# Routing into fixed visits: an expert's first 512 tokens keep their own visit, one-hot rows are built column by column, and the first visit is transposed tile by tile

## What is computed

```python
def _moe_ref(x, w_gate, w_noise, noise, w1, w2):      # N, D, E, F = 1536, 320, 8, 1024
    logits = x @ w_gate
    noise_scale = np.log1p(np.exp(x @ w_noise))
    noisy_logits = logits + noise_scale * noise
    top2 = np.argpartition(-noisy_logits, 2, axis=1)[:, :2]
    ...                                                # top2_w: softmax over the two
    for e in range(E):
        for k in range(2):
            mask = top2[:, k] == e
            h = np.maximum(x[mask] @ w1[e], 0.0)
            out[mask] += top2_w[mask, k, None] * (h @ w2[e])
```

## Time and profile before

| | before |
|---|---|
| median of 3 runs | 757.9 us |
| lowest, highest | 757.38, 763.17 us |
| profiled execution | 757.65 us |
| its span, first to last instruction | 755.5 us |
| mean granted clock of PE | 0.955 of full |
| PE busy | 680.6 us, 90% |
| DVE, ACT, POOL busy | 400.1, 286.8, 107.8 us |
| `h_hi` steps (line 545) | 160: 20 visits of 8 steps, 8 in layer 1, 12 in layer 2 |

### The profile page before, as it was taken

How to read it: one execution, slowest core, us unless ns; L and a number is a source line. 1 busy time by engine, 2 the same in 40 slices (tenths; PEclk the granted TensorE clock), 3 DMA queues, 4 the chain that set the end, 5 groups by cost and what they waited for, 6 DMA issues and landing times.

```text
span 755.5 us, 11010 instructions
## 1 busy us (share of the span) xinstructions
PE 680.6 (90%) x4020; PEld 610.9 (81%) x4021; DVE 400.1 (53%) x615; ACT 286.8 (38%) x466; POOL 107.8 (14%) x134
## 2 busy tenths in 40 slices
PE   2999953598999999999739999999999999999997
PEld 2889722598899898898638899898888888889887
DVE  7677549565445465365335545554554554444522
ACT  6644250245444354354214343343342332333311
POOL 4333204710201201200060200101200001000000
PEclk9999885699999999999959999999999999999999
DMA  7667660775445455450146352443432423513000
GB/s 209 147 146 171 191 242 10 196 225 156 150 122 153 131 161 159 127 158 35 37 153 189 105 154 63 126 126 107 144 97 84 125 83 108 150 60 95 0 0 35
DMA packets 32565, 93.11 MB, mean 123 GB/s; under 512 B 4848, under 2 KB 14832, under 8 KB 32528
## 3 DMA queue, kind: packets, MB, share of 16 engines
q1 hardware_dynamic: 25040, 76.23, 34.8%
q0 software_dynamic: 3264, 11.15, 5.6%
q10 hardware_dynamic: 4224, 5.24, 1.9%
HBM read 79.49 MB, written 13.11 MB: 123 GB/s over the span
## 4 chain that ended last, share of the span: by engine, by line
PE 86%; DVE 7%; issue 2%; DMA 2%; ACT 1%; POOL 1%; DVEq 0%; ACTq 0%; POOLq 0%
PE pY L1073 12%; PE pY L1074 12%; PE pY L1075 12%; PE pH L1060 10%; PE pH L1061 9%; PE pH L1062 9%; PE pH L1065 5%; PE pH L1063 5%; PE psS L918 3%; PE psYa L971 3%; PE pT L1041 2%; PE psYa L984 1%; PE psF L1005 1%; PE psD L928 1%; PE pT L1042 1%
## 5 line engine op out<-in xcount | busy, mean ns | idle before, releaser
L545 ACT ACTIVATE h_hi<-pH 128x512 fp32r<-128x512 f32 x160 | 95.8, 599 | 292.9 <-PE pH L1065 292.9
L811 DVE SCALAR_TENSOR_TENSOR h_lo<-pH,h_hi 128x512 fp32r<-128x512 f32 x160 | 110.5, 691 | 177.2 <-ACT h_hi L545 176.1
L1073 PE MATMUL pY<-w_hi,h_hi 128*128 128x320 f32 x608 | 188.9, 311 | 3.0 <-DVE h_lo L811 2.6
L1074 PE MATMUL pY<-w_lo,h_hi 128*128 128x320 f32 x608 | 187.5, 308 | 0.0
L1075 PE MATMUL pY<-w_hi,h_lo 128*128 128x320 f32 x608 | 187.5, 308 | 0.0
L1060 PE MATMUL pH<-x_hi,w_hi 128*128 128x512 f32 (+2 forms) x324 | 128.4, 396 | 9.2 <-issue 5.7
L1061 PE MATMUL pH<-x_lo,w_hi 128*128 128x512 f32 (+2 forms) x324 | 124.7, 385 | 0.0
L1062 PE MATMUL pH<-x_hi,w_lo 128*128 128x512 f32 (+2 forms) x324 | 124.2, 383 | 0.0
L1073 PEld LDWEIGHTS pY<-w_hi,h_hi 128*128 128x128 f32 x608 | 114.1, 188 | 12.1 <-issue 5.7
L645 DVE TENSOR_TENSOR w_lo<-stage,w_hi 128x1024 fp32r<-128x1024 f32 (+1 forms) x80 | 108.5, 1358 | 25.6 <-ACT w_hi L491 25.5
L1074 PEld LDWEIGHTS pY<-w_lo,h_hi 128*128 128x128 f32 x608 | 114.1, 188 | 4.2
(11 more groups left out here) (184 smaller groups left out, 625.5 us busy)
## 6 DMA issues: line engine op xcount, KB each, us to landing
stage<-in_w SPq DMA_DIRECT2D x40, 640.0 KB, 3.9
stage<-in_w SPq DMA_DIRECT2D x40, 512.0 KB, 3.6
stage<-in_w SPq DMA_DIRECT2D x40, 256.0 KB, 3.9
results_by_slot<-acc ACTq DMA_DIRECT2D x8, 640.0 KB, 3.7
qk<-in_qk_t SPq DMA_DIRECT2D x16, 240.0 KB
kv<-in_kv_n SPq DMA_DIRECT2D x8, 480.0 KB
results_by_slot<-acc SPq DMA_DIRECT2D x6, 640.0 KB, 9.4
og<-in_o_n SPq DMA_DIRECT2D x2, 960.0 KB, 9.4
```

Of the source, the lines that this page charges most:

```text
L545: act.activation(HH[s % 2][:, :], pH[s % 2][:, :], ACT.Relu).then_inc(hh_done[layer], 1)
L811: dve.scalar_tensor_tensor(out=HL[s % 2][:, :], in0=pH[s % 2][:, :], scalar=0.0, in1=f32(HH[s % 2][:, :]), op0=ALU.max, op1=ALU.subtract). ...
L1073: pe.matmul(y[:, 0:XD], hh, wh, start=(f == 0), stop=False)
L1074: pe.matmul(y[:, 0:XD], hh, wl, start=False, stop=False)
```

## The change

- **Fixed visits.** Expert e's first 512 tokens go to visit e. Only what exceeds 512 goes to spare visits (`OVER` = 6 of them). Every choice gets a position `at` = 2048 e + rank (`SPAN`), and e x 2048 enters by a third matmul (`bases`) added to `psU`. The plan of the spare visits, and `rowid` for them, `dest` and the counts, are computed after the first 8 visits' `rowid`.
- **Tile and place.** `hi`, the tile's first position, is `at` rounded by adding and subtracting a large number; `lo` is the rest.
- **One-hot by column.** For each of the 24 columns DVE makes `in_row` (128 elements) and the tile-id half of `ids` (32 elements), with a scalar per lane; POOL makes the other half (32 elements) likewise. PE sums groups of 4.
- **Spare visits.** 24 more matmuls (`psO`, 48 columns) give the spare visits' rows. They stand in PE's queue behind the first tile's transposes and wait for `over_picked`.
- **First visit.** Each tile of it has a semaphore (`xin_first`) and is transposed as it lands, into six banks in two halves; ACT and DVE work by halves, and `up` of the first step waits for each round by itself.
- **Weights.** ACT's first `split_hi` moves ahead of its `xT` copies, DVE's `split_lo` of pieces 0 to 3 ahead of the logits; piece 4 stays behind `rowid`. SP loads the weights of visits 1 to 7 by a fixed number. Seven matmuls of 512 columns replace the 32 of 128 whose results nobody reads.

```diff
-            pool.wait_ge(rt_reached, 1)
-            for k in range(2):
-                ...
-                    pool.tensor_tensor(reached_id[:, at, n, :], reached[:, at, :], ...
+            pool.wait_ge(rt_where, 1)
+            for n in range(2 * NT):
+                pool.tensor_scalar(ids[:, n, 1, :], row_of[:, :, :].rearrange("p e t -> p (e t)"), hi[:, n // NT, n % NT:n % NT + 1], lane[:, 0:1],
+                                   ALU.is_equal, ALU.mult).then_inc(rt_lanes, 1)
 ...
+            split_hi(0, 0, 0, range(PIECES))
             for t in range(1, NT, 2):
 ...
             act.activation(e2[:, :], dl[:, :], ACT.Exp).then_inc(rt_e2, 1)
-            split_hi(0, 0, 0, range(PIECES))
 ...
+            split_lo(0, 0, 0, (0, 1, 2, 3))
             dve.wait_ge(rt_ln, 1)
 ...
+            rlink(dve.tensor_tensor_scan(line(incl), reset96[:, :], psU, 0.0, ALU.mult, ALU.add))
+            rlink(dve.tensor_tensor(line(pos), psR, line(incl), ALU.add))
+            for k in range(2):
+                ins = dve.tensor_tensor(d8[:, k, :, :], oh[:, k, :, :], pos[:, :, :].rearrange("p e t -> p t e"), ALU.mult)
+            rlink(ins)
 ...
+            rlink(dve.tensor_reduce(flat24(at), d8[:, :, :, :].rearrange("p k t e -> p (k t) e"), AX.X, ALU.add))
+            rlink(dve.tensor_scalar(flat24(hi), flat24(at), -(P - 1) / 2, TO_TILE, ALU.add, ALU.add))
+            rlink(dve.tensor_scalar(flat24(hi), flat24(hi), TO_TILE, None, ALU.subtract))
+            rlink(dve.tensor_tensor(flat24(lo), flat24(at), flat24(hi), ALU.subtract))
+            dve.sem_inc(rt_where, 1)
+            for n in range(2 * NT):
+                k, t = n // NT, n % NT
+                dve.tensor_scalar(in_row[:, n, :], iotaP[:, :], lo[:, k, t:t + 1], None, ALU.is_equal)
+                dve.tensor_scalar(ids[:, n, 0, :], row_of[:, :, :].rearrange("p e t -> p (e t)"), hi[:, k, t:t + 1], float(t),
+                                  ALU.is_equal, ALU.mult).then_inc(rt_place, 1)
+            dve.wait_ge(rt_inv, 1)
+            rlink(dve.tensor_copy(part[:, :], psI[:, MR:2 * MR]))
+            dve.scalar_tensor_tensor(out=rowid[:, 0:MR], in0=psI[:, 0:MR], scalar=float(P), in1=part[:, :], op0=ALU.mult, op1=ALU.add).then_inc(rt_rows, 1)
+            split_lo(0, 0, 0, (4,))
 ...
+            dve.tensor_scalar(over_ids[:, :, 1, :], over_in[:, :, :], lane[:, 0:1], None, ALU.mult).then_inc(over_picked, 1)
 ...
-            pe.matmul(psU, ones[:, :], rows, start=True, stop=True).then_inc(rt_rank, 1)
+            pe.matmul(psU, ones[:, :], rows, start=True, stop=False)
+            pe.matmul(psU, ones[:, :], bases[:, :], start=False, stop=True).then_inc(rt_rank, 1)
 
             for n in range(2 * NT):
                 if n % INV == 0:
-                    pe.wait_ge(rt_place, n // INV + 1)
-                if n % NT == 0:
-                    pe.wait_ge(rt_tokens, n // NT * 2 + 2)
 ...
+                    pe.wait_ge(rt_place, n + INV)
+                    pe.wait_ge(rt_lanes, n + INV)
+                ins = pe.matmul(psI[:, 0:2 * MR], in_row[:, n, :], ids[:, n, :, :].rearrange("p n r -> p (n r)"), start=(n == 0), stop=(n == 2 * NT - 1))
 ...
+            for bank in (*pH, pY[3], *pH, *pH):
+                pe.matmul(bank[:, :], iotaP[:, :], keep_busy, start=True, stop=True)
 ...
+            for half in range(2):
+                for n in range(2):
+                    tt = 2 * half + n
+                    pe.wait_ge(xin_first[tt], 16)
+                    for k in range(3):
+                        if k == 2 and half == 1 and n == 0:
+                            pe.wait_ge(over_rows, 1)
+                        ins = turn(pF[half][k][:, n * P:(n + 1) * P], xrows[0][:, tt, :], k)
+                        if n == 1:
+                            ins.then_inc(tr_mm[0], 1)
+                    if tt == 0:
+                        pe.wait_ge(over_picked, 1)
+                        for m in range(2 * NT):
+                            ins = pe.matmul(psO[:, 0:2 * OVER * ST], in_row[:, m, :], over_ids[:, m, :, :].rearrange("p n r -> p (n r)"),
+                                            start=(m == 0), stop=(m == 2 * NT - 1))
+                        ins.then_inc(over_inv, 1)
+            pe.wait_ge(rt_tiles, 2)
```

More of the change, by code:

```diff
@@ L49 @@
 RB = 4
-INV = 6
+INV = 4
+OVER = V1 - MUST
+MR = MUST * ST
+SPAN = 2048
+TO_TILE = 1.5 * 2 ** 23 * P
 NEG = -1.0e30
@@ L99, in build @@
         dest = sb("dest", [P, 2, NT], U32)
[L100 to L104, removed]
+        eid = sb("eid", [1, OVER + 1], I32)
+        tiles = sb("tiles", [1, E1], I32)
+        in_use = sb("in_use", [1, OVER])
         counts = sb("counts", [1, 1], I32)
@@ L192, in build @@
         rt = ExitStack()
[L193 to L196, removed]
+        turned = ExitStack()
+        xT = sb("xT", [P, 3, N], F32, turned)
+        flat = sb("flat", [2 * E1, N], F32, turned)
+        turned.close()
+        over_in = sb("over_in", [P, 2 * NT, OVER * ST], F32, rt)
+        over_ids = sb("over_ids", [P, 2 * NT, 2, OVER * ST], BF16, rt)
@@ L197, in build @@
+        in_row = sb("in_row", [P, 2 * NT, P], BF16, rt)
+        ids = sb("ids", [P, 2 * NT, 2, MR], BF16, rt)
+        ez, sc, lg, mx, t8 = (
+            sb(n, [P, NT, E1], F32, rt) for n in ("ez", "sc", "lg", "mx", "t8"))
         ix = sb("ix", [P, NT, E1], U32, rt)
-        ixf = sb("ixf", [P, NT, 2], F32, rt)
+        ixf = sb("ixf", [P, 2, NT], F32, rt)
         dl, e2, s2 = (sb(n, [P, NT], F32, rt) for n in ("dl", "e2", "s2"))
-        A, incl, tot, excl, pos = (sb(n, [P, E1, NT], F32, rt) for n in ("A", "incl", "tot", "excl", "pos"))
@@ L201, in build @@
-        over = sb("over", [P, E1, N // SLOT], F32, rt)
-        sl0, slots, sincl, sexcl = (sb(n, [P, E1], F32, rt) for n in ("sl0", "slots", "sincl", "sexcl"))
-        df, hi_part = (sb(n, [P, 2 * NT], F32, rt) for n in ("df", "hi_part"))
-        lo_part = sb("lo_part", [P, 2 * NT], BF16, rt)
-        reached = sb("reached", [P, 2 * NT, RT + 1], BF16, rt)
-        reached_id = sb("reached_id", [P, 2 * NT, 2, RT + 1], BF16, rt)
-        in_row = sb("in_row", [P, 2 * NT, P], BF16, rt)
-        row_ids = sb("row_ids", [P, 2, RT], F32, rt)
@@ L209, in build @@
-        past = sb("past", [1, SLOTS + 1, E1], F32, rt)
-        ef = sb("ef", [1, SLOTS + 1], F32, rt)
+        A, incl, pos = (sb(n, [P, E1, NT], F32, rt) for n in ("A", "incl", "pos"))
+        oh, d8 = (sb(n, [P, 2, NT, E1], F32, rt) for n in ("oh", "d8"))
+        at, lo, hi, rank, late, shift = (sb(n, [P, 2, NT], F32, rt) for n in ("at", "lo", "hi", "rank", "late", "shift"))
+        over = sb("over", [P, E1, N // SLOT - 1], F32, rt)
+        more, oincl, oexcl, delta = (sb(n, [P, E1], F32, rt) for n in ("more", "oincl", "oexcl", "delta"))
@@ L738, in _ @@
             dve.wait_ge(rt_rank, 1)
-            rlink(dve.tensor_copy(tot[:, :, :], psU.rearrange("p (e t) -> p e t", e=E1)))
             line = lambda x: x[:, :, :].rearrange("p e t -> p (e t)")
-            rlink(dve.tensor_tensor_scan(line(incl), reset96[:, :], line(tot), 0.0, ALU.mult, ALU.add))
-            rlink(dve.tensor_tensor(excl[:, :, :], incl[:, :, :], tot[:, :, :], ALU.subtract))
-            rlink(dve.tensor_tensor(pos[:, :, :], psR.rearrange("p (e t) -> p e t", e=E1), excl[:, :, :], ALU.add))
```

247 lines of the change are left out of this document (141 added, 106 removed).

## The result

The changed kernel took 754.86 us (median of 16 executions, 750.00 to 759.39), the kernel before in the same measurement 758.98 (16, 755.09 to 763.17). The ratio is 0.9943, 95% interval 0.9917 to 0.9969: 4.3 us gained where 9.2 were forecast, outside the range of 744.8 to 753.3. The profiled execution took 750.60 us, its span 748.8.

The account below looks back on a forecast made before the run. TensorE is busy 90%, mostly with unchanged dense matmul, so only the router's slack-free chain of waits could pay. Gains 6.0 + 2.3 + 0.9 = 9.2 us from 757.9 gave 748.7; range for 8 in 10: 744.8 to 753.3.

Parts of the forecast that it names:

- Up to the one-hot work: Router before the one-hot operations: they start at 114.4 where in_row started at 120.2, a gain of 5.8 us.
- the new run of DVE work: Router, from incl to the first one-hot operation: DVE's new short operations take 2.3 us.
- DVE's pairs: Router one-hot work on DVE: 24 pairs of 128 and 32 elements at 0.28 us each, 6.7 us.
- POOL's 24 operations: Router, other half of ids: 24 operations of 32 elements at 0.25 us, 6.0 us, just inside DVE's time.
- T: End of rowid in the router, 128.31 us before the change; forecast 122.3, a gain of 6.0.
- My first rival: Router one-hot work: small operations pay their full fixed part, pair 0.48 or POOL 0.45; gain 4.4, 753.5 us; chance 0.2.
- its tail of 2.3: From the end of rowid to visit 0's first matmul: gain 2.3 us, between 0.9 and 3.5.
- The moved work: ACT's weight copies and DVE's first four splits, moved into idle time ahead of the router: cost nothing.
- From T on: From the end of rowid to visit 0's first matmul: 14.0 us instead of 16.3, gain 2.3.
- the overflow matmuls: PE's 24 matmuls for spare visits, before visit 0: 0.138 us each, 3.3 us at the low clock.
- The clock: Start of visit 0: 3.66 us of low-clock work may take 1.83; even odds, so 0.9 us gained.
- visit 1's low clock: Start of visit 1, granted 0.54 after 2.2 us of idle: argument against a high clock at visit 0.

Follow-up runs that it names:

- ids_dve: Changed kernel, with the ids rows made on DVE by three operations over all 24 columns and none on POOL: 749.49 us, ratio 0.9893.
- again2: The changed kernel, not a byte different, measured again in a later set: 749.58 us, ratio 0.9903.
- sp_head: Changed kernel plus one already-true wait on SP, behind its wait for attention's end, 20 us ahead of the stretch: 750.38 us, ratio 0.9904.
- before2: The kernel before, unchanged, measured and profiled again: 755.92 us, ratio 1.000.
- again: The changed kernel, same bytes, measured again in the first set for a second profile: 755.56 us, ratio 0.9970.

## Why the forecast was wrong, step by step

**Up to the one-hot work: right.** The third `psU` matmul cost 0.44, the new run of DVE work 2.3, and the start came 4.49 after A (forecast 4.36). Of the 5.8 forecast, 5.7 were gained.

**DVE's pairs: slightly small.** 0.317 for 0.28, 7.6 us for 6.7. The elements counted for less than I made them: 32 and 128 elements cost nearly the same, 0.15 and 0.166. The Trainium skill (VectorE: DVE Perf Modes, section "The TRN2 errata") has a fixed latency for each instruction and the advice to use tiles of 512 elements or more; the trace agrees on the fixed part. My estimate of 0.17 for a pair took that page's 58 cycles and is half of what was measured; the same section says that 58 is too few and that some 150 were measured, by which a pair is an estimated 0.36 at the page's 0.96 GHz, nearer the 0.317 here.

**POOL's 24 operations: the step that failed.** "I take 0.25, 6.0 us, just inside DVE's." They took 0.474 each, 11.4 in all, and became the bound: T came 4.6 us later than the sum had it, 3.5 of them POOL's by the estimate under `ids_dve`. The bounds were there, 0.19 and 0.61, and I took the value by size (32 elements are near 16) from a row of another kind, a select without a scalar per lane. My first rival names POOL at 0.45 and gives T a gain of 1.2; measured are 1.4 (18.27 less 16.86). That rival, at 0.2, is right about POOL and wrong about DVE, whose pairs it had at 0.48. PE's waits above show POOL as the bound in every group, and with the `ids` work made wide T is 5.2 earlier (`ids_dve`). That the rival's total, 4.4 and 753.5, lies close to the 4.3 and 754.86 on record is luck: its tail of 2.3 did not come there.

**The moved work: right.** DVE's four splits ended 0.2 us before ACT's `sc` released `t` (0.3 forecast); ACT's copies ended at 84.3, before its first `xT` at 86.15; from the first transpose to A it took 22.45 against 22.62.

**From T on: the place was right, the size was not.** In the sets without the stall the first `pH` matmul is at T + 12.64 to T + 12.85 (ten kernels that keep the order of PE's work); I had T + 14.0, between 12.7 and 15.4. The term that was too big is the overflow matmuls: 24 took 1.14 us at the low clock, not 3.3. I priced them by the 0.138 of the `psF` matmuls, and both halves of that were wrong. The 2.49 us for 18 hold two waits between groups; inside a group they start 0.095 apart. And they have 114 columns, these 48: 0.095 x 48 / 114 is 0.040, and 0.040 apart is how these start. The fourth gather's issue began at T + 5.3 (5.0), tile 3 was there at T + 9.0 to T + 9.4 in the kernels without the stall (8.6), `over_picked` at T + 6.8 (7.1). On record, the stall of 3.8 ate this gain of 3.6 whole: T + 16.55, -0.3. I had no term for it, and could not have: `again2` shows the same program without it.

**The clock: the right stretch, too much by half, and another left out.** The 1.2 GHz stretch at visit 0's start shrank from 3.83 to 2.84 us (windows of the changed kernel):

```profile
141.16:144.00 2.84, 2.84 (x9) 2.84 (x10) 0.00 (x0) 0.00 (x0) 2.23 (x3) 0.50 1.08 241
```

Half of such a stretch is lost, so 0.5 us were won; I had 0.9. But I had used visit 1's low clock, granted 0.54 in its first 3.4 us, only as an argument. It is in both profiles of the kernel before and in none of the three of the changed kernel:

```profile
169.22:172.62 3.40, 3.20 (x17) 2.89 (x18) 0.82 (x2) 1.71 (x3) 0.00 (x0) 1.00 0.60 205
```

Half of it is 1.7 us. The ten kernels without the stall that keep the order of PE's work don't all gain it: eight have that stretch, `again2` and `sp_head` have not. From the first `pH` matmul to the end of the span it is 610.9, 609.0 (`before2`), 607.7 (changed), 609.0 (`again`) and 607.4 us (`again2`), with 27.7, 25.4, 20.6, 25.3 and 20.3 us of that at 1.2 GHz. Less half of the latter, 596.3 to 597.4 remain in all five: behind that matmul single profiles differ by their clock and by little else.

**The sum.** On record: 1.4 - 0.3 + 0.5 = 1.6, and the repetition `again` gives 2.3 (0.8 to 3.7). The 4.3 on record has an interval of 2.4 to 6.3, and the 16 executions of before beside it had a median 2.6 to 3.3 above those of the later sets; what lies between 1.6 and 4.3 is not accounted for by the stretch that was changed. The term that failed most is POOL's, 4.6 at T; the stall took 2.6 more between forecast and record (-0.3 for 2.3), and its cause stays open. Where there is no stall: 1.4 + 3.6 + 0.5 = 5.5 against 7.3 (5.5 to 9.2) for `again2`. Visit 1's 1.7 would close that gap, which three profiles can't prove of a median. The 749.58 of `again2` lies in the range and 0.9 from the forecast; that would have been luck, with T 4.6 later after A than the sum had it. The forecast of 9.2 exceeds 5.5 by the one-hot work (4.6 at T) and the clock (0.4), less what the tail was better (1.3).

## What to carry to other kernels

A list of small operations dealt out to two engines costs what the slower engine asks for an instruction, so price the second engine by a row of its own with the same kind of operands, or don't use it; three wide operations in place of 48 small ones were worth 5 us. Price matmuls by columns, not by count, and from a run of them that has no wait inside. And when an edit makes a stall vanish, run a control that changes the program as little and the order not at all, and the unchanged kernel beside it: two edits here seemed to prove a cause, and the controls and then the unchanged kernel lost the stall as well.

## What the runs showed that was not expected

- POOL: 0.474 us for a two-step operation of 32 elements with scalars per lane, 3.02 for one step on 768; DVE's operations of 128 elements beside the latter went from 0.166 to 0.21 apart.
- DVE: unlinked operations with a scalar per lane are 0.15 to 0.17 apart for 32 and for 128 elements alike, while each is listed with 0.23 to 0.25.
- TensorE's first branch inside the loop: 0.38 us where a fetch of 16 KB stands ahead of it, 3.57 where the fetch stands inside it, 7.22 in the set with the stall. Fewer instructions ahead of the loop made the entry dearer, not cheaper.
- A state of a whole set of measurements, seen with and without it on one chip, in which TensorE's increments reach the other engines up to 4 us late, instructions of SP take 0.7 us, records of landings are missing, and the changed kernel loses 4 us, the kernel before 1.6. Its cause stays open.
- A dip of the clock to 1.2 GHz for 6.8 us at the end of attention that comes or stays away with the moment at which the clock first rose, 2.1 us in a single profile: two profiles must be aligned at the edit, not at their start.
